# A linear-attention and two-layer expert kernel: heads moved to partitions 0 and 64, with another split of the work among the engines

## The reference

```python
for t in range(S):                     # S = 768, D = 48
    kt, vt, rt = (k[:, :, t], v[:, :, t], r[:, :, t])
    cur = np.einsum('bhd,bhe->bhde', u[None] * kt, vt)
    y[:, :, t] = np.einsum('bhd,bhde->bhe', rt, state + cur)
    state = w[None, :, :, None] * state + np.einsum('bhd,bhe->bhde', kt, vt)
...
# x: 3072 tokens of 384 features; each token goes to one of 8 experts of 384 tokens,
# in the order of the gate logits x @ w_gate
for e in range(E):
    mask = assigned == e
    h = np.maximum(x[mask] @ w1[e], 0.0)      # 384 -> 1024
    out[mask] = h @ w2[e]                     # 1024 -> 384
...
h = np.maximum(x @ w_in, 0.0)                 # 384 -> 2048
return (h * h @ w_out)                        # 2048 -> 384
```

## Time and profile before

| | us |
|---|---|
| median of 3 runs | 917.77 (915.58 to 920.63) |
| span of the profiled execution, first to last instruction | 916.4 |
| first scores matmul starts, in the profile | 17.19 |
| last `yrow` ends | 192.9 |

### The profile page before, as it was taken

The page is one execution under the profiler, slowest core; times in us unless marked ns, Lnnn a source line. Parts: engine busy times, 40 slices in busy tenths (PEclk is TensorE's granted clock), DMA queues, the critical chain, the costliest instruction groups (busy, mean ns, idle before and its releaser), DMA issues.

```text
span 916.4 us, 17340 instructions
## 1 busy us (share of the span) xinstructions
PE 844.8 (92%) x6216; PEld 813.4 (89%) x6216; DVE 568.5 (62%) x1159; ACT 277.6 (30%) x506; POOL 357.5 (39%) x338
## 2 busy tenths in 40 slices
PE   2999899953599999999999999999999999999995
PEld 2999899952489998999999899989999999999995
DVE  6998989867558645845683586459456832851210
ACT  0112212111204521541253145315422532542331
POOL 4887878731203520531153035205411531442233
PEclk9988989875699999999999999999999999999998
DMA  4565656402201200300130022003100400220000
GB/s 158 180 212 184 210 181 218 162 20 70 94 1 71 95 26 0 131 32 26 41 122 7 19 69 94 26 0 104 59 26 17 146 0 26 95 70 26 1 1 26
DMA packets 21741, 69.82 MB, mean 76 GB/s; under 512 B 3152, under 2 KB 6352, under 8 KB 21712
## 3 DMA queue, kind: packets, MB, share of 16 engines
q1 hardware_dynamic: 18640, 59.99, 19.7%
q0 software_dynamic: 3072, 9.44, 2.9%
HBM read 59.98 MB, written 9.44 MB: 76 GB/s over the span
## 4 chain that ended last, share of the span: by engine, by line
PE 73%; DVE 3%; POOL 3%; issue 2%; ACT 0%; DMA 0%; POOLq 0%; DVEq 0%; ACTq 0%
PE bank L1104 16%; PE bank L1106 14%; PE bank L1105 14%; PE bank L1158 7%; PE bank L1160 7%; PE bank L1159 7%; PE bank L1051 4%; PE bank L1084 1%; DVE hot L806 1%; PE bank L1057 1%; POOL rku L384 1%; POOL state L398 1%; POOL kn L395 1%; PE bank L1073 1%; DVE hot L717 0%
## 5 line engine op out<-in xcount | busy, mean ns | idle before, releaser
L441 POOL TENSOR_TENSOR h_lo<-sq,h_hi 128x384 fp32r<-128x384 f32 x128 | 152.9, 1198 | 410.1 <-DVE sq L881 410.0
L881 DVE SCALAR_TENSOR_TENSOR sq<-bank,relu 128x384 f32<-128x384 f32 x128 | 71.1, 556 | 132.9 <-ACT relu L509 132.8
L1158 PE MATMUL bank<-m_hi,h_hi 128*128 128x384 f32 x384 | 131.6, 343 | 0.0
L1104 PE MATMUL bank<-x_hi,m_hi 128*128 128x384 f32 x384 | 130.6, 340 | 0.3
L1160 PE MATMUL bank<-m_hi,h_lo 128*128 128x384 f32 x384 | 128.6, 335 | 0.0
L1106 PE MATMUL bank<-x_hi,m_lo 128*128 128x384 f32 x384 | 128.6, 335 | 0.0
L1159 PE MATMUL bank<-m_lo,h_hi 128*128 128x384 f32 x384 | 128.5, 335 | 0.0
L1105 PE MATMUL bank<-x_lo,m_hi 128*128 128x384 f32 x384 | 128.4, 334 | 0.0
L509 ACT ACTIVATE relu<-bank 128x384 f32<-128x384 f32 x128 | 63.0, 492 | 194.4 <-PE bank L1106 194.1
L503 ACT ACTIVATE h_hi<-bank 128x384 fp32r<-128x384 f32 x64 | 31.5, 492 | 202.4 <-PE bank L1106 202.4
L873 DVE SCALAR_TENSOR_TENSOR h_lo<-bank,h_hi 128x384 fp32r<-128x384 f32 x64 | 35.5, 554 | 71.9 <-ACT h_hi L503 71.9
(11 more groups left out here) (170 smaller groups left out, 1712.0 us busy)
## 6 DMA issues: line engine op xcount, KB each, us to landing
w_raw<-we_in SPq DMA_DIRECT2D x48, 512.0 KB, 4.9
nn<-nn_in SPq DMA_DIRECT2D x24, 576.0 KB, 3.9
tt<-tt_in SPq DMA_DIRECT2D x24, 384.0 KB, 3.3
m_raw<-m_in SPq DMA_DIRECT2D x12, 512.0 KB, 5.2
x_rows<-yrow SPq DMA_DIRECT2D x24, 192.0 KB, 1.9
xg<-x_rows,perm_next POOLq DMA_INDIRECT x24, 4.7
out<-xg,perm_now POOLq DMA_INDIRECT x24, 2.6
u_row<-u_in SPq DMA_DIRECT2D x1, 192.0 KB, 3.0
```

The costliest lines, as they stand in the source:

```text
L441: pool.tensor_tensor(h_lo[g % 3][:, :], sq[g % 2][:, :], h_hi[g % 3][:, :].bitcast(f32), ALU.subtract).then_inc(lo2_ready, 1)
L881: dve.scalar_tensor_tensor(out=sq[g % 2][:, :], in0=h_ps[g % 3][:, 0:CAP], scalar=0.0, in1=relu[:, :], op0=ALU.max, op1=ALU.mult).then_inc ...
L1104: pe.matmul(out, hi_w, hi_x, start=first, stop=False)
L1158: pe.matmul(acc_ps[t][:, 0:DM], h_hi[r][:, s], m2_hi[:, c:c + DM], start=first, stop=False)
```

## The change

It concerns the attention alone, and the tables in front of it.

- **Layout.** The first head of a pair lies on partitions 0 to 47 and the second on 64 to 111 (`HALF = 64`, `HD = 112`); the 16 partitions between hold zeros or ones, set once at the start. `kb` with its two masked copies becomes `ks` with one, and `kpow_b`, `pairmask` and `decay` go.
- **TensorE.** Scores are again 8 matmuls (L1043), each over its own head's 48 rows, 0 to 47 or 64 to 111 in turn. The product with the state becomes 8 such matmuls with 48 columns (L1052) where 4 with 96 rows and 96 columns stood. `update` becomes 8 matmuls of 48x48 (L1065) that write partitions 0 to 47 or 64 to 111. The 8 products with the masked scores stay (L1075). The state is 112x192 instead of 96x384.
- **Division of work.** The own term `ownv` goes from one GpSimd instruction to 8 on ScalarE (L508, one a head, each with a per-partition factor), and the decay from one on GpSimd to 4 on ScalarE (L517).
- **Order and buffers.** `tt` and `nn` have four buffers, one a sequence, `am` has two; `y_ps` has two banks for each of its two buffers. TensorE's order in a unit is `front(n+1)` with the state product in it, `turn(n-1)`, `back(n)`, `gate(n-1)`, `state_update(n+1)`. VectorE masks the next unit and scales the one after it before it makes the rows of this one. The last four units skip the state update.
- **Loads.** `tt` comes in two transfers of 48 partitions instead of one of 96, each unit three units earlier than before relative to its use.

```diff
@@ sizes and buffers
+HALF = 64
+HD = HALF + D
...
-        tt = [sb(f"tt{j}", [PD, 2, PAIRS, P], f32, att) for j in range(2)]
-        nn = [sb(f"nn{j}", [P, 3, DM], f32, att) for j in range(2)]
...
-        kb = sb("kb", [PD, PAIRS, 2, P], f32, att)
+        tt = [sb(f"tt{b}", [HD, 2, PAIRS, P], f32, att) for b in range(B)]
+        nn = [sb(f"nn{b}", [P, 3, DM], f32, att) for b in range(B)]
...
+        ks = sb("ks", [HD, PAIRS, P], f32, att)
...
-        am = sb("am", [P, 2, 512], f32, att)
-        zt = sb("zt", [PD, PAIRS, PD], f32, att)
-        state = [sb(f"state{b}", [PD, PAIRS, PD], f32, att) for b in range(B)]
+        am = [sb(f"am{j}", [P, 2, 512], f32, att) for j in range(2)]
+        zt = sb("zt", [HD, PAIRS, D], f32, att)
+        state = [sb(f"state{b}", [HD, PAIRS, D], f32, att) for b in range(B)]
...
@@ GpSimd, one unit: ownv and the decay leave, kn comes first
-                    pool.tensor_tensor(ownv[j][:, :].rearrange("p (h d) -> p h d", h=H),
...
-                    pool.tensor_tensor(state[b][:, :, :], zt[:, :, :], decay[:, :, :, :].rearrange("p q a d -> p q (a d)"),
...
+                        updates(i + (b + 1) // B, (b + 1) % B)
+                    bonus(i + (b + 1) // B, (b + 1) % B)
@@ ScalarE, one unit
+                    for h in range(H):
+                        cols = slice(h * D, (h + 1) * D)
+                        done = act.activation(ownv[j][:, cols], nn[b][:, 2, cols], ACT.Copy, scale=own[j][:, h:h + 1])
+                    done.then_inc(ownv_ready, 1)
+                    if not is_first(n):
+                        turned_y(n - 1)
+                    if not last:
+
+                        act.wait_ge(z_ready, n + 1)
+                        act.wait_ge(inter_done, n + 1)
+                        for p in range(PAIRS):
+                            done = act.activation(state[b][:, p, :], zt[:, p, :], ACT.Copy, scale=w_chunk[:, p:p + 1])
+                        done.then_inc(state_ready, 1)
+                    if not is_first(n):
+                        gated(n - 1)
+                    if b % 2 and not (last and b == B - 1):
+                        m2_high(2 * i + b // 2 + 1, 1 - b // 2, i + 1 + b // 2)
@@ VectorE: table and scaling
-            tab(dve.tensor_tensor(kpow_b[:, :, :, :], kpow[:, :, :].unsqueeze(2).broadcast_to([PD, PAIRS, 2, P]),
...
-            tab(dve.tensor_tensor(decay[:, :, :, :], w_chunk[:, :].unsqueeze(2).unsqueeze(3).broadcast_to([PD, PAIRS, 2, D]),
...
+                dve.tensor_tensor(ks[:, :, :], tt[b][:, 1, :, :], kpow[:, :, :], ALU.mult)
+                dve.tensor_tensor(rs[b % 2][:, :, :], tt[b][:, 0, :, :], powr[:, :, 0:P], ALU.mult).then_inc(scaled, 1)
@@ VectorE, one unit
+                    if not last or b < B - 1:
+                        mask(*one)
+                    if not last or b < B - 2:
+                        scale(*two)
+                    rows(i, b)
+                    if not last or b < B - 1:
+                        own_sum(*one)
+                    if not last:
+                        state_sum(*one)
+                    m2_low(i, b)
@@ TensorE
+                for p in range(PAIRS):
+                    for a in range(2):
+                        rows = slice(a * HALF, a * HALF + D)
+                        last = pe.matmul(sc_ps[a][:, p * P:(p + 1) * P], ks[rows, p, :], rs[j][rows, p, :], start=True, stop=True)
...
+                    for a in range(2):
+                        rows = slice(a * HALF, a * HALF + D)
+                        last = pe.matmul(y_ps[j][:, a, p * D:(p + 1) * D], rs[j][rows, p, :], state[b][rows, p, :],
+                                         start=p == 0, stop=False)
...
+                for p in range(PAIRS):
+                    for a in range(2):
+                        c = slice((2 * p + a) * D, (2 * p + a + 1) * D)
+                        last = pe.matmul(u_ps[a * HALF:a * HALF + D, p * D:(p + 1) * D], kn[:, c], nn[b][:, 2, c], start=True, stop=True)
...
+                        last = pe.matmul(y_ps[j][:, a, p * D:(p + 1) * D], am[j][:, a, p * P:(p + 1) * P], nn[b][:, 2, c],
+                                         start=False, stop=p == PAIRS - 1)
...
+                    if not end:
+                        front(i + (b + 1) // B, (b + 1) % B)
+                    if not is_first(n):
+                        turn(n - 1, (b - 1) % B)
                     back(i, b)
+                    if not is_first(n):
+                        gate(n - 1)
+                    if not last:
                         state_update(i + (b + 1) // B, (b + 1) % B)
```

More of the change, by code:

```diff
@@ L401, in _ @@
-            with pool.Fori(0, NC - 1) as i:
+                    if last and b == B - 1:
+                        continue
+                    if last:
+                        pool.wait_ge(nn_in[b + 1], 16 * i + 16)
+                    else:
+                        updates(i + (b + 1) // B, (b + 1) % B)
+                    bonus(i + (b + 1) // B, (b + 1) % B)
+            pool.wait_ge(table, N_TABLE)
+            updates(0, 0)
+            bonus(0, 0)
+            units(0, False)
+            with pool.Fori(1, NC - 1) as i:
@@ L482, in split_high @@
+            m2_high(0, 0, 1)
+            units(0, False)
+            with act.Fori(1, NC - 1) as i:
+                units(i, False)
+            units(NC - 1, True)
+            turned_y(NU - 1)
+            gated(NU - 1)
             def split_high(q, j):
@@ new lines, in own_sum, with state_sum @@
+            def own_sum(i, b):
+                n, j = 4 * i + b, b % 2
+                dve.wait_ge(rku_ready, n + 1)
+                if not (isinstance(n, int) and n < 2):
+                    dve.wait_ge(ownv_ready, n - 1)
+                dve.tensor_reduce(own[j][:, :], rku[j][:, :].rearrange("p (h d) -> p h d", h=H), AX.X,
+                                  ALU.add).then_inc(own_ready, 1)
+            def state_sum(i, b):
+                n = 4 * i + b
+                dve.wait_ge(state_ready, n + B)
+                dve.wait_ge(update_ready, n + 1)
+                dve.tensor_tensor(zt[:, :, :], state[b][:, :, :],
+                                  u_ps[0:HD, 0:PAIRS * D].rearrange("p (q f) -> p q f", q=PAIRS), ALU.add).then_inc(z_ready, 1)
@@ L623, in _ @@
+                    m2_low(i, b)
+            tabbed()
             for b in range(B):
                 dve.sem_inc(y_stored[b], 16)
-            with dve.Fori(0, NC - 1) as i:
+            scale(0, 0)
+            mask(0, 0)
+            scale(0, 1)
+            own_sum(0, 0)
+            state_sum(0, 0)
+            units(0, False)
+            with dve.Fori(1, NC - 1) as i:
                 units(i, False)
@@ L961, in scores @@
                 last.then_inc(scores_ready, 1)
-            def update(j):
+                pe.wait_ge(state_ready, n + 1)
+                if not (isinstance(n, int) and n < 2):
+                    pe.wait_ge(y_ready, n - 1)
                 for p in range(PAIRS):
-                    c = slice(p * PD, (p + 1) * PD)
-                    last = pe.matmul(u_ps[0:PD, c], kn[:, c], nn[j][:, 2, c], start=True, stop=True)
-                last.then_inc(update_ready, 1)
-            def gate(n):
-                pe.wait_ge(yT_ready, n + 1)
-                if not is_first(n):
-                    pe.wait_ge(logit_ready, n)
-                for d in range(DC):
-                    last = pe.matmul(lg_ps[:, 0:E], yT[:, d * P:(d + 1) * P], wg[:, d, :], start=d == 0, stop=d == DC - 1)
-                last.then_inc(logit_sum, 1)
@@ L1043, in _ @@
             units(NC - 1, True)
+            turn(NU - 1, B - 1)
             gate(NU - 1)
```

285 lines of the change are left out of this document (135 added, 150 removed).

## The result

The changed kernel takes 971.4 us (median of 4 runs, 971.38 to 971.45) against 918.07 before: a ratio of 1.056, with a 95% interval of 1.053 to 1.060. It is 53 us slower; I had forecast 891, a gain of 26.

The account below looks back on a forecast made before the run. GpSimd's instruction chain bound the old attention; TensorE would bind the new at 5.80 us a unit, 135.5 at full clock, 150.5 at 0.90. Attention ending 26 us earlier gave 890 span, 891 us median; range 878 to 938.

Parts of the forecast that it names:

- I take 0.90, which makes 150.5: Attention stage: TensorE's 135.5 us at full clock divided by an assumed mean clock of 0.90 gives 150.5 us.
- Rival 2: Attention: passes overlap, but the clock is at 1.2 GHz for half the stage (mean 0.75), giving 922 us; chance 0.12.
- no waits are left: TensorE in the attention: nothing should be waited for, the argument against the clock staying low for much longer.
- Row groups side by side: Scores and state product: passes on partitions 0 to 47 and 64 to 111 overlap, 1.78 us a unit for 32 passes.
- Rival 1: Scores and state product: row groups follow one another, 3.55 us for 32 passes, 932 us in all; chance 0.28.
- The sum at full clock: TensorE's attention unit: 2.79 unchanged products + 0.78 update + 1.78 scores and state + 0.45 shape changes = 5.80 us.
- The three changes of shape: TensorE, each unit: into and out of the 48-row products and into the 48-column update, 0.15 us each, 0.45 together.
- rival 3: Attention: VectorE or ScalarE binds; at VectorE's upper 6.4 us a unit the stage takes 154, giving 895 us; chance 0.10.
- The ring: Attention: five GpSimd instructions and a VectorE reply set the old unit, 7.2 us; the change takes this apart.
- the hindered end: VectorE's attention work while GpSimd also multiplies out of SBUF: `ks` and `rs` 1.27 us each, `m2_lo` 1.06.
- GpSimd's upper bound of 3.9 us: GpSimd per attention unit: `kn`, `rk` and `rku` remain, 0.95 + 0.96 + 1.0 to 1.6, given as 2.9 to 3.9 us.
- The first scores: Start of the attention: moves from 17.19 to about 14.8 us, with bounds of 0.5 and 4 on the gain.

Follow-up runs that it names:

- the run of 899.1: Changed kernel plus dense matmuls before the first scores and four matmuls a unit that compute nothing, between transposes and masked product: 899.1 us against 917.3 for the kernel before.
- the isolated mix of the kernel before: A kernel without the computation: six units of the previous kernel's product mix, after some 13 us of TensorE rest; no kernel time given, clock low throughout.
- warm start: Changed kernel plus dense 128-row, 128-column matmuls in TensorE's idle time before the first scores: 971.3 us.
- the 910.85 beside 892.6: One of five executions of the changed kernel with state product over all rows, dense matmuls before the first scores and three idle matmuls a unit; the version took 892.9 us.
- the block run: A kernel without the computation: 60 dense matmuls, then 14 units of the changed kernel's mix without waits, three matmuls replacing the transposes; no kernel time given.

## Why the prediction was wrong

**What fell.** The failing step is the clock: "I take 0.90, which makes 150.5". The clock was 0.50 for the whole stage, from 16.72 to 245.9 us. I had divided TensorE's work by the mean of before, as if it belonged to the kernel, but it belongs to the mix of passes. By the sum's own terms, 135.5 us at full clock are 271 at 0.50; the stage took 229, since the terms were high (below): a unit at the low clock takes 9.72 us, less than twice the forecast's 5.80. Rival 2 had the mechanism, "the new passes stream 48 columns in 48 rows", but with half of the stage low and a chance of 0.12. What I put against it, "no waits are left", was no protection: TensorE was busy for 228.6 of 229.2 us at 1.2 GHz. The Trainium skill, page "TensorE: Matmul & The Clock Gate", section "Why this matters for your kernels", advises to keep TensorE busy without a break, which is to bring the high clock. Here TensorE was busy without a break and had the low one, and the measurement decides against the advice for this mix.

**Row groups side by side: right.** Forecast 16 scores passes in 0.9 us; at high clock they took 1.00 (49.75 to 50.75) and the state product 0.92, at low clock 1.87 and 1.71. Rival 1 (0.111 for each pass) is out. Of the two pages that the prediction cites, the Trainium skill's "TensorEngine Tiling (Array Packing)", section "Key Properties", is borne out: different tiles load and multiply in parallel. The Trainium skill's "TensorE: Matmul & The Clock Gate", section "LDWEIGHTS", says that a load's time goes by its columns and not by its rows. The trace agrees for a single load, since one group of 48 rows kept 16 passes in 3 us, as 128 rows did at that clock; but two such loads run at once, and so it doesn't lead to rival 1.

**The sum at full clock: 5.80 against 5.26.** Scores and state product 1.92 (forecast 1.78), masked product and gate 1.72 + 0.73 = 2.45 (2.45), transposes 0.39 (0.34), update 0.50 (0.78, with a lower bound of 0.40). The three changes of shape, 0.45, are within these figures: at the start of the scores above, the second pair comes 0.21 us behind the first and each later one 0.11, so about 0.1 for this change and not 0.15. Whether a full clock would have given 24 x 5.26 isn't shown, for VectorE comes close: it was busy 32.3 us of the 40 from 27 on with four extra ahead of the scores, 5.1 a unit, and 36.7 to 37.1 of each 40 in the run of 899.1, 5.7 a unit. I had taken 5.5 for it. At 5.7 it, and not TensorE, would set the pace (rival 3), close to the 5.80 of my sum.

**The ring: right.** With the clock mostly restored by undoing the two products, order and division of work gave 21 us, a unit of 6.0 to 6.1 against 7.32. `kn` waits for the update and no longer the reverse. `ks` and `rs` averaged 0.90 and 0.75 us against 1.27 at the hindered end, and `rku` 1.04 against 1.62: GpSimd and VectorE overlap less. Part of that is the longer unit, though: in the run of 899.1, at the high clock, `rs` and `rku` stay at 0.80 and 1.06, but `ks` averages 1.32. (GpSimd's upper bound of 3.9 us is mis-added, 0.95 + 0.96 + 1.6 is 3.5; it doesn't bind either way.)

**Small terms.** A ScalarE copy of 48 columns shows 320 ns, but eight lie within 1.91 us, 0.23 each, near the 0.21 taken. The first scores came at 16.72, not 14.8: `ks` and `rs` at the start took 1.19 and 1.48 while GpSimd ran `kn` and `rk`, so the gain was 0.5, the lower bound. Routing and experts behind the attention kept their time: 53 us late at 245.9, 53 late at the end.

**What stays open.** How much each product contributes was only bracketed: each alone left the clock falling, both undone held it. Why the isolated mix of the kernel before stays low for 65 us, while the kernel itself mostly runs high, is open. That the block starts from rest isn't the reason by itself, for in the kernel before the clock also rises from low, at 22.5 us and again after each of its falls in the attention (behind 3.4 or 6.8 us). The block differs from the kernel in having no transposes, no waits and another order of the scores. And no version of the changed kernel was run at a held high clock without extra matmuls, so its time there isn't known.

## What to carry to other kernels

Before cheaper passes are bought on TensorE, ask what they do to its clock: halving the time of the only products with long streams can leave a mix that runs at 1.2 GHz with the engine fully busy. Read the clock from the distance of passes of a known form, not from the clock's row alone. Where a stage sits at the edge, the place and the number of a few idle matmuls decide: four a unit in the light stretch gave 899.1 us against 971.4 without them, three a unit without a warm start 1002.2. Such a stage can also fall back in single executions, as the 910.85 beside 892.6 shows.

## What the runs showed of the hardware

- Before a trace's first recorded change the clock reads 1.00, at whatever level it is: 308 passes in the same 40 us at a recorded 1.00 and 0.50.
- Two float32 passes over partitions 0 to 47 and 64 to 111, with weights of 128 columns each, start 3 to 7 ns apart, and pairs follow each other after 0.112 us at the high clock, so 0.056 each: their weight loads overlap too.
- Passes of 128 rows that stream 48 columns, or of 96 rows that stream 96, don't raise the clock in 41 us without a gap; passes of 128 rows with 48 weight columns that stream 48, in pairs, do within 7.
- Idle matmuls of 128 rows and 128 columns in the light stretch of this kernel: four a unit raised a low clock (at 38 us) and it stayed high for 126 us; three a unit without a warm start left it low throughout. In the block run, without waits and transposes, three a unit held a high clock for 14 units.
